# Attention of a fused attention, mixture-of-experts and gated feed-forward kernel: output rows turned by VectorE, query growth multiplied in at the PSUM read, first residents loaded and split late

## The reference, cut to what matters

```python
def _attn_ref(q, k, v):                       # 4 batches, 8 heads, 768 steps, head size 64
    gamma = 1.0 - 2.0 ** (-5.0 - np.arange(H))
    scale = 1.0 / np.sqrt(D)
    for t in range(S):
        state = gamma * state + outer(k[:, :, t], v[:, :, t])
        y[:, :, t] = scale * (q[:, :, t] @ state)

x = attn_out.transpose(0, 2, 1, 3).reshape(3072, 512)
x = _moe_ref(x, ...)     # each of 8 experts takes 384 rows, greedily by logits = x @ w_gate
return _moe2_ref(x, ...) # (sigmoid(x @ w_gate) * (x @ w_val)) @ w_out, inner size 1536
```

## Time and profile before

| | |
|---|---|
| median of 3 runs | 1087.48 us (1087.31 to 1087.81) |
| the profiled execution | 1085.66 us, its span 1083.8 us |
| TensorE busy in the span | 95% |
| VectorE, ScalarE, GpSimd busy | 62%, 32%, 12% |
| TensorE in the chain that ended last | 95% |
| DMA issues in the attention | q, k, v: 24 each of 256 KB; rows: 24 of 256 KB |

### The profile page before, as it was taken

The page is one execution under the profiler, slowest core; times in us unless marked ns, Lnnn a source line. Parts: engine busy times, 40 slices in busy tenths (PEclk is TensorE's granted clock), DMA queues, the critical chain, the costliest instruction groups (busy, mean ns, idle before and its releaser), DMA issues.

```text
span 1083.8 us, 19943 instructions
## 1 busy us (share of the span) xinstructions
PE 1029.3 (95%) x7130; PEld 960.1 (89%) x7130; DVE 673.1 (62%) x1853; ACT 346.2 (32%) x659; POOL 128.5 (12%) x157
## 2 busy tenths in 40 slices
PE   6999933999999999999999999999999999999996
PEld 5888823999999999999999999999999999999995
DVE  3545468877577657766676677756775677554211
ACT  3444433422333233322332333223412342234110
POOL 4544401033010101010100010011001100110001
PEclk9999965999999999999999999999999999999998
DMA  9999443313241324122321332142314231323000
GB/s 225 252 238 229 129 136 113 113 39 88 78 137 49 89 78 127 60 77 89 108 79 56 110 104 83 49 117 90 97 40 127 79 108 36 120 78 118 1 1 29
DMA packets 186986, 107.65 MB, mean 99 GB/s; under 512 B 80785, under 2 KB 169361, under 8 KB 186897
## 3 DMA queue, kind: packets, MB, share of 16 engines
q1 hardware_dynamic: 183056, 93.94, 30.7%
q0 software_dynamic: 3840, 12.59, 3.6%
HBM read 88.41 MB, written 18.09 MB: 98 GB/s over the span
## 4 chain that ended last, share of the span: by engine, by line
PE 95%; DVE 3%; DMA 1%; issue 1%; SPq 0%; POOL 0%; ACT 0%; DVEq 0%; POOLq 0%
PE bank L1294 21%; PE bank L1296 21%; PE bank L1295 21%; PE bank L1387 6%; PE bank L1388 6%; PE bank L1386 6%; PE bank L664 3%; PE bank L641 2%; PE bank L637 2%; PE bank L598 1%; PE bank L1248 1%; PE bank L605 1%; PE bank L616 1%; PE bank L651 1%; PE bank L622 1%; PE bank L589 1%
## 5 line engine op out<-in xcount | busy, mean ns | idle before, releaser
L1294 PE MATMUL bank<-h2h,resident 128*128 128x384 f32 x768 | 261.2, 340 | 0.0
L1296 PE MATMUL bank<-h2h,resident 128*128 128x384 f32 x768 | 257.9, 336 | 0.0
L1295 PE MATMUL bank<-h2l,resident 128*128 128x384 f32 x768 | 257.3, 335 | 0.0
L1294 PEld LDWEIGHTS bank<-h2h,resident 128*128 128x128 f32 x768 | 144.4, 188 | 3.0
L1295 PEld LDWEIGHTS bank<-h2l,resident 128*128 128x128 f32 x768 | 144.3, 188 | 2.9
L1296 PEld LDWEIGHTS bank<-h2h,resident 128*128 128x128 f32 x768 | 144.1, 188 | 0.0
L805 ACT ACTIVATE ring<-ring_raw 128x512 fp32r<-128x512 f32 x192 | 117.6, 623 | 62.7 <-DMA ring_raw<-in_moe_w_out_dram 40.5
L829 ACT ACTIVATE ph<-pf 128x384 fp32r<-128x384 f32 x96 | 50.4, 525 | 252.5 <-DVE pf L1121 252.5
L1121 DVE TENSOR_TENSOR pf<-bank,gate 128x384 f32<-128x384 f32 x96 | 53.5, 557 | 123.6 <-PE bank L1296 115.8
L1130 DVE TENSOR_TENSOR ring<-ring_raw,ring 128x512 fp32r<-128x512 f32 x192 | 126.0, 682 | 0.0
L825 ACT ACTIVATE gate<-bank 128x384 f32<-128x384 f32 x96 | 46.9, 489 | 146.3 <-PE bank L1296 146.2
(11 more groups left out here) (192 smaller groups left out, 1661.8 us busy)
## 6 DMA issues: line engine op xcount, KB each, us to landing
ring_raw<-in_moe_w_dram SPq DMA_DIRECT2D x128, 256.0 KB, 3.1
ring_raw<-in_moe_w_out_dram SPq DMA_DIRECT2D x64, 256.0 KB, 2.8
qraw<-in_q_dram SPq DMA_DIRECT2D x24, 256.0 KB, 3.6
kraw<-in_k_dram SPq DMA_DIRECT2D x24, 256.0 KB, 4.0
vraw<-in_v_dram SPq DMA_DIRECT2D x24, 256.0 KB, 4.3
xrows<-xrow SPq DMA_DIRECT2D x24, 256.0 KB, 2.3
xlaid<-xg SPq DMA_DIRECT2D x7, 768.0 KB, 4.3
zg<-xlaid SPq DMA_DIRECT2D x28, 192.0 KB, 4.2
```

What stands on the lines that cost most here:

```text
L1294: nc.tensor.matmul(ps, wh, xhi, start=start, stop=False)
L1295: nc.tensor.matmul(ps, wh, xlo, start=False, stop=False)
L1296: return nc.tensor.matmul(ps, wl, xhi, start=False, stop=stop)
```

## The change

Five edits, all in the attention.

- Queries are no longer scaled: TensorE transposes `qraw` itself. A new table `growth` holds scale * gamma^t in y's layout. It is made once at the start by 48 products of TensorE, and copied out of PSUM by three instructions of ScalarE and three of VectorE. VectorE multiplies it in while it reads y from PSUM (`xTa`).
- `xTa` is turned to rows by VectorE, in 32x32 blocks, straight into `xrow`. TensorE's four transposes and ScalarE's copy go. The blocks leave the rows of a unit in an order that takes four stores, each from 32 partitions with pieces of 512 bytes.
- TensorE makes the scores right behind the logits, at the head of the slot; VectorE updates the state behind the mask and behind `xTa`.
- q, k and v have semaphores of their own. q of unit u+6 is loaded as soon as q of unit u is transposed, k as soon as `ks` of unit u is made, v after unit u's state update.
- The sixteen early residents are loaded in slots 19 to 22, four in each, with the high part on ScalarE in slots 21 to 26 (three in a slot) and the low part on GpSimd behind its last `ks`. Seven residents share memory with the attention in place of four.

```diff
-        shared = at_big + (RESIDENT - 4) * 2 * 512 * 4
+        shared = at_big + (RESIDENT - SHARED) * 2 * 512 * 4      # SHARED = 7
+        def high(act, r):
+            if r % GROUPED == 0:
+                act.wait_ge(resident_loaded[r // GROUPED], 16 * GROUPED)
+            nc.scalar.activation(resident[:, r, 0, :], resident_raw[r][:, :], ACT.Copy).then_inc(resident_hi, 1)
...
                 def store(u):
...
+                    for j in range(QUADS):
+                        sp.dma_start(xrows[u * P:(u + 1) * P, j * P:(j + 1) * P].rearrange("(t i) x -> i t x", i=QUAD),
+                                     xrow[j * QUAD:(j + 1) * QUAD, c, :].rearrange("i (t x) -> i t x", x=P)).then_inc(xrow_stored[c], 16)
...
+                    if s >= U - C + 1 and group < EARLY // GROUPED:
+                        for r in range(group * GROUPED, (group + 1) * GROUPED):
+                            load_resident(sp, r)
...
             def attend_scalar(act):
...
-                        nc.scalar.activation(xrow[:, cc, :], ps_x[:, :], ACT.Copy).then_inc(xrow_ready, 1)
...
-                        nc.scalar.activation(xTa[:, cc % 2, :, :], ps_y[:, :].rearrange("p (a t) -> p a t", a=KD),
-                                             ACT.Copy, scale=SCALE).then_inc(xT_ready, 1)
+                    if s is not None and s >= U - C + 3:
+                        while highs[0] < min(EARLY, 3 * (s - U + C - 2)):
+                            high(act, highs[0])
+                            highs[0] += 1
...
             def attend_vector(dve):
...
-                        nc.vector.tensor_tensor(qs[:, c % 2, :, :], qraw[:, c, :, :],
-                                                dec[:, 0, c, :].unsqueeze(2).to_broadcast([P, H, D]),
-                                                ALU.mult).then_inc(qs_ready, 1)
+                    if alive(s, 4):
...
+                        nc.vector.transpose(xrow[:, cc, :].rearrange("p (t j a) -> p a t j", j=QUAD, a=KD),
+                                            xTa[:, cc % 2, :, :].rearrange("p a (t i) -> p a t i", i=QUAD)).then_inc(xrow_ready, 1)
...
+                        nc.vector.tensor_tensor(xTa[:, cc % 2, :, :], ps_y[:, :].rearrange("p (a t) -> p a t", a=KD),
+                                                growth[:, cc, :, :], ALU.mult).then_inc(xT_ready, 1)
...
             def attend_tensor(pe):
...
+                for c in range(C):
+                    for a in range(NPAIR):
+                        for half in range(2):
+                            last = nc.tensor.matmul(grown_in[c][half * D:half * D + D, a * P:(a + 1) * P],
+                                                    dec[:, 0, c, 2 * a + half:2 * a + half + 1].to_broadcast([P, D]), ident[:, :],
+                                                    start=True, stop=True)
+                    last.then_inc(growth_turned, 1)
...
-                        for a in range(KD):
-                            last = nc.tensor.transpose(ps_x[:, a:DM:KD],
-                                                       xTa[:, cc % 2, a, :], ident[:, :])
-                        last.then_inc(x_transposed, 1)
```

## The result

The changed kernel takes 1081.99 us (median; its runs go from 1079.96 to 1084.76) against 1087.48 (1087.31 to 1087.98): a ratio of 0.9949 [0.9938, 0.996]. It is faster, by 5.5 us where I had said 17.5, and 1082 lies outside 1066 to 1077. The profiled execution is the longest of its five, 1084.76 with a span of 1082.7, so its rows tell of a gain of 1.1 us of span, not 5.5.

What follows compares the result with a forecast made beforehand. The prediction took TensorE to bound the attention, busy for 105.80 of 105.80 us. Gains of 12.8 (slots), 1.9 (start) and 2.8 (end) sum to 17.5, so 1087.48 becomes 1070.0 us, range 1066 to 1077.

Steps and rivals of the forecast that it cites:

- The slots: Attention, 20 slots from slot 5 to 25: mean slot 4.65 us in place of 5.29, a gain of 12.8 us.
- No wait, so a full slot is 4.85: Attention slot: the 0.17 us wait put down to VectorE's logits' copy would not recur, so removing x's transposes saves 0.64.
- The start: Before slot 5, with the table's 48 products: slot 5 starts at 22.8 us, a gain of 1.9 (0.3 to 4.4).
- The end: From slot 25 to the last logits' copy: 9.2 us in place of 12.0, a gain of 2.8.
- The residents: Loads in slots 19 to 22: the last lands about one slot late, hidden before ScalarE needs it in slot 25.
- the issues have room: SyncE's queue in the attention: seven issues a slot in place of four fit, as q and k are asked for earlier.
- The rival of the last quarter: Attention's last quarter: residents over two slots late, or low parts running into the route, give 1075 us; chance 0.09.
- The sum: Whole kernel: gains of 12.8, 1.9 and 2.8 us make 17.5, so 1070.0 us from the median.
- The rounds only move: Behind the attention: the route of 45 us and the rounds come earlier and are otherwise unchanged.
- T: Time of VectorE's turn of `xTa` in each slot: 1.12 us, hidden up to 1.72.
- the quarters of a store: Attention's DMA: four transfers of 1.05 us, 4.2 a slot against 4.65; the rival that they hold the queue had 0.03.
- the row on `zg`: Rounds' loads in four transfers from or to 32 partitions: 4.2 us for 1.05 MB, used to price a store at 1.05.

Runs made afterwards that it cites:

- e1: The changed kernel with TensorE making the logits behind the scores in place of ahead of them; 1082.61 us, ratio 0.9953 to the kernel before.
- e7: The changed kernel with the four stores issued by ScalarE and the logits behind the scores; 1075.22 us, ratio 0.9891 to the kernel before.
- e2: The changed kernel with ScalarE's 16 early high parts made behind the attention; 1091.91 us, ratio 1.0038 to the kernel before.
- e11: The changed kernel with high parts behind the attention and GpSimd's low parts behind the first gather; 1097.32 us, ratio 1.0091 to the kernel before.
- e3: The changed kernel with each unit stored by one transfer of whole rows, output not the reference's; 1078.19 us, ratio 0.9906 to the kernel before.

## Why the prediction was wrong

The direction was right and the size was not: 5.5 of 17.5 us. The sum had three terms; a fourth belonged in it.

- **The slots: 12.8 forecast, 6.8 measured.** The step that failed is "No wait, so a full slot is 4.85". I had asked whether VectorE could cause the wait of 0.17 anew, and it could not; but it had not caused it before either. The wait stands before the 32-column weights in every order tried. So the transposes were worth 0.47, which the text had as its lower bound. The reorder, which I had costed at nothing, takes back about 0.13, of which e1 shows 0.10 to be the logits' place. The full slot is 5.15 for 5.49, and 20 slots without the stall take 99.0 for 105.8.
- **The start: 1.9 forecast, 2.2 measured.** Slot 5's logits come at 22.52 for 24.70. The 48 products for the table take 6.7 us (2.68 to 9.33), inside 5.1 to 9.2. There is luck in this term: with the same products the other ten kernels begin slot 5 at 22.63 to 24.05 us, and their table takes 6.8 to 8.3. Their gains of 0.7 to 2.1 are mostly below the forecast.
- **The end: 2.8 forecast, 1.6 measured.** From slot 25 to the last copy's end it is 10.36 us for 12.0, not 9.2. Most of it is slot 26: my chain had a wait of 1.1 and y, 2.8 us, and the slot takes 3.73 (133.25 to 136.98), as its logits and parts stand in it too. TensorE's wait of 1.09 there is for VectorE's logits' copy, which stands behind the state update.
- **The residents: "Hidden" forecast, 7.5 us lost.** The step that failed is "the issues have room". I had counted seven issues in place of four and priced the stores by their bytes alone, never their time on SyncE, which the trace of before has rows for. A round of SyncE's loop takes 4.4 to 4.8 us where the slot is 4.93, so the lag from its first loads is hardly made up. The rival of the last quarter had this mechanism, and nearly the size: residents more than two slots late, one slot more worth "up to 4.65". They were three slots late, which cost 5.4 in the gap and 2.1 in the slot at half speed. Slot 25 comes at 129.06, and without the stall it would at 22.52 + 99.01 = 121.53.
- **The sum** 6.8 + 2.2 + 1.6 - 7.5 = 3.1 is what the last copy moved (142.48 to 139.42, ends). Of it 2.0 goes again in the profiled execution: 0.3 in the route, and 1.7 in the rounds, of which the first starts with a granted clock of 0.82 in 182.19 to 193.20, where it was 1.00 before. "The rounds only move" did not hold there.
- **Right:** T at 1.12; VectorE and the turn hidden in the full slots; TensorE without a gap up to the stall, so the kernel was TensorE's and not the queue's; the quarters of a store. For those the Trainium skill (DMA: Bandwidth & Descriptors, Bandwidth) would have made an estimated slot of 6.95, by its 0.95 us for 64 KB. Four quarters take 2.59 us of SyncE and the slot is 5.15, so here the row on `zg` was the better guide.

Had e7 been the change, the forecast would have missed by 5.2. By its rows the last copy falls 5.5 short: 4.1 in the slots (97.1 us, where 12.8 less than 105.8 was forecast), 1.5 in the end, less 0.2 that the start gained.

Open: why the runs of the change spread over 5 us and those of before over 0.7. Each kernel has rows for one execution only. Across the kernels three stretches vary that no edit explains: the start of slot 5 (22.52 to 24.05), the stall where there is one (7.5, 5.8 and 4.0), and the granted clock in the first 11 us of the rounds. With 1.00 there the rounds take 898.7 to 899.2 us, with 0.82 to 0.84 they take 900.3 to 900.5, with 0.74 to 0.78 they take 900.9 to 901.9. What makes these three vary is not shown. Also open is why low parts stretch many VectorE instructions by one of theirs in e2 and hold one through all sixteen in e11.

## What to carry to other kernels

When a change gives a queue more instructions, add up their issue time on the engine that issues them, not only their bytes, and ask by how many steps that engine lags already: what stands at the queue's end is late by the whole lag. A wait with a releaser beside it is only that releaser's if it goes when the releaser moves; where it recurs before the same shape whatever stands ahead, take it as part of the instruction. A wait inside an in-order engine's body costs all that is queued behind it, so a load that is not urgent must be asked for well before the engine comes to it.

## What the runs showed of the hardware

- Four stores of 64 KB from 32 partitions take 2.0 to 3.6 us of SyncE's queue in the change, one store of the same 256 KB from 128 partitions 0.6 to 1.4 in e3.
- A series of 16 GpSimd subtractions (1.2 us each) holds one VectorE instruction of 0.25 us for 19.99.
- Successive VectorE turns overlap: 1.13 us long, 0.98 from start to start.
- A change to 32-column weights shows 0.17 us in TensorE's row, in each slot looked at, whether the transposes of x or those of k stood before it.
- After a gap of 5.48 us TensorE's granted clock was 0.50 for 4.4 us (scores' loads 1.79 for 0.97).
- Sixteen low parts on GpSimd in the attention cost TensorE nothing (20 slots of 99.01 us with and without them); in the route they cost 12 us.
